# A third staging buffer, a new order of VectorE's additions, and residual additions on GpSimd, in a fused attention and mixer kernel

## The reference

```python
x  = attention(q, k, v)             # 4 batches, 576 tokens, 8 heads x 64, window 128
u  = x + (x^T @ U @ V)^T            # tokens mixed through rank 32: "the mixed tokens"
x2 = u + relu(u @ w_ch1) @ w_ch2    # w_ch1 512x2048, w_ch2 2048x512
# then a gated unit: relu(x2 @ w_in), layer norm, spatial product, gate, @ w_out
```

## Time and profile before

| what | value |
|---|---|
| median of 3 runs | 742.33 us (742.27 to 743.06) |
| the profiled execution | 742.42 us |
| its span, first to last instruction | 740.6 us |
| TensorE matmul busy | 719.5 us, 97% of the span |
| weight load busy | 664.1 us, 90% |
| VectorE busy | 457.0 us, 62% |
| ScalarE busy | 339.2 us, 46% |
| GpSimd busy | 182.0 us, 25% |

### The profile page before, as it was taken

How to read it: one execution, slowest core, us unless ns; L and a number is a source line. 1 busy time by engine, 2 the same in 40 slices (tenths; PEclk the granted TensorE clock), 3 DMA queues, 4 the chain that set the end, 5 groups by cost and what they waited for, 6 DMA issues and landing times.

```text
span 740.6 us, 13178 instructions
## 1 busy us (share of the span) xinstructions
PE 719.5 (97%) x4688; PEld 664.1 (90%) x4688; DVE 457.0 (62%) x1032; ACT 339.2 (46%) x764; POOL 182.0 (25%) x183
## 2 busy tenths in 40 slices
PE   7999999999999999989899999999999999999998
PEld 5777777689989989989799999999899998998997
DVE  6878787788763365226977885986365435444331
ACT  5977777854452243224344444445262432432422
POOL 1597546520007873353041000000010100100100
PEclk9999999999999999999999999999999999999999
DMA  6569954046446864798976454667820100100101
GB/s 207 185 232 394 336 207 136 16 150 206 170 147 239 285 248 164 233 385 312 428 253 195 146 166 136 193 222 264 304 108 1 54 12 0 64 0 0 64 0 65
DMA packets 74066, 128.24 MB, mean 173 GB/s; under 512 B 5024, under 2 KB 44960, under 8 KB 73504
## 3 DMA queue, kind: packets, MB, share of 16 engines
q1 hardware_dynamic: 74016, 127.59, 49.4%
HBM read 76.91 MB, written 50.66 MB: 172 GB/s over the span
## 4 chain that ended last, share of the span: by engine, by line
PE 61%; DVE 8%; DMA 4%; issue 3%; POOL 2%; ACT 1%; SPq 0%; DVEq 0%; POOLq 0%; ACTq 0%
PE bank L1881 5%; PE bank L1883 5%; PE bank L1882 5%; PE bank L1923 4%; PE bank L1925 4%; PE bank L1924 4%; PE bank L2032 2%; PE bank L2034 2%; PE bank L2033 2%; PE bank L1846 2%; PE bank L1848 2%; PE bank L1847 2%; PE wide L1847 2%; PE wide L1846 2%; PE wide L1848 2%
## 5 line engine op out<-in xcount | busy, mean ns | idle before, releaser
L1881 PE MATMUL bank<-xs,w1s 128*128 128x384 f32 x336 | 114.2, 340 | 7.4 <-DVE tok L1414 4.0
L1883 PE MATMUL bank<-xs,w1s 128*128 128x384 f32 x336 | 113.0, 336 | 0.0
L1882 PE MATMUL bank<-xs,w1s 128*128 128x384 f32 x336 | 113.0, 336 | 0.0
L1055 ACT ACTIVATE rk<-tok 128x768 fp32r<-128x768 f32 x72 | 60.8, 848 | 77.8 <-PE bank L1925 35.6
L901 POOL TENSOR_TENSOR vl<-vr,vh 128x512 fp32r<-128x512 f32 x8 | 11.3, 1407 | 293.5 <-ACT vh L1179 293.5
L1038 ACT ACTIVATE sums_u<-bank 128x384 f32<-128x384 f32 x72 | 35.4, 492 | 99.2 <-PE bank L1883 90.1
L914 ACT ACTIVATE sc<-sc,mn 128x256 f32<-128x256 f32 (+1 forms) x144 | 67.0, 468 | 20.4 <-DVE mn L1239 20.3
L1923 PE MATMUL bank<-rk,w2q 128*128 128x384 f32 x208 | 70.5, 339 | 4.0 <-DVE rk L1436 2.3
L1881 PEld LDWEIGHTS bank<-xs,w1s 128*128 128x128 f32 x336 | 63.5, 189 | 10.4 <-DVE tok L1414 5.3
L1924 PE MATMUL bank<-rk,w2q 128*128 128x384 f32 x208 | 69.5, 334 | 0.0
L1925 PE MATMUL bank<-rk,w2q 128*128 128x384 f32 x208 | 69.5, 334 | 0.0
(11 more groups left out here) (220 smaller groups left out, 1847.8 us busy)
## 6 DMA issues: line engine op xcount, KB each, us to landing
r_scr<-tok SPq DMA_DIRECT2D x18, 768.0 KB, 4.3
tok<-r_scr SPq DMA_DIRECT2D x18, 768.0 KB, 7.6
qkraw<-qk SPq DMA_DIRECT2D x32, 288.0 KB, 4.0
w1raw<-w SPq DMA_DIRECT2D x32, 256.0 KB, 3.6
w2q<-w_scr SPq DMA_DIRECT2D x4, 2048.0 KB, 13.9
wc_scr<-wprep SPq DMA_DIRECT2D x12, 512.0 KB, 6.0
w_scr<-tok SPq DMA_DIRECT2D x11, 512.0 KB, 2.8
u_scr<-tok SPq DMA_DIRECT2D x6, 768.0 KB, 4.4
```

The source lines that it names most:

```text
L1055: act.activation(rk[:, n % RING, 0], raw(g, RAW_OF[m])[:, 2 * j:2 * j + 2, :], ACT.Relu if m <= 3 else ACT.Copy).then_inc(rk_hi, 1)
L1881: pe.matmul(o, wh, ah, start=(k == 0 and m in FRESH), stop=False, skip_group_check=True)
L1882: pe.matmul(o, wl, ah, start=False, stop=False, skip_group_check=True)
L1883: last = pe.matmul(o, wh, al, start=False, stop=(k == 1), skip_group_check=True)
```

## The change

Six edits, all in the second stage:

1. Step 22 stages its blocks in a new buffer `late2`, with a semaphore `r_last` of its own for its store, and waits for no earlier store. `late2` covers the third slot of the ring `rk`, so `hi_r(2)` waits for `r_last` and moves behind the last `keep_p`. The load of `raw_c` no longer waits for the store of step 22. Steps 18 to 21 and 23 use `late0` and `late1` as before.
2. At a change of group `c12(s-1)` goes ahead of `x_sum(g+1, 2)` and of the low parts 5 and 7; `c11` and `c22` of the last step change places; ScalarE does `hi_xs(g+1, 1)` ahead of `c21`, and `hi_xs(g, 7)` after `hi_xs(g, 5)`; `X_ORDER` has 5 ahead of 7. `relu_b(s-1)` now stands behind `lo_xs(g, 5)` and `lo_xs(g, 7)` in step u = 0.
3. At the start `c22(0)` goes ahead of `w1_sum_of(2)` (four additions of 128x256).
4. In `SUMS[0]` the sums (3,0) and (2,0) move up to entry (1,3), and the rest follows by one place.
5. `add_res` moves from VectorE to GpSimd, for all groups, in one loop that stands behind `split_direct(4)`.
6. `dc21` of groups 0 and 1 is done two entries later.

```diff
-X_ORDER = [1, 2, 6, 7, 5, 4, 3]
+X_ORDER = [1, 2, 6, 5, 7, 4, 3]
...
+LATE_AT = {18: 0, 19: 1, 20: 0, 21: 1, 22: 2, 23: 1}
...
-    0: {(2, 0): [(3, 0), (2, 0)], (2, 1): [(3, 1), (2, 1)], (2, 2): [(3, 2), (2, 2)], (2, 3): [(3, 3), (2, 3)],
-        (6, 0): [(4, 0), (1, 0)], (6, 1): [(4, 1), (1, 1)], (6, 2): [(4, 2), (1, 2)], (6, 3): [(4, 3), (1, 3)]},
+    0: {(1, 3): [(3, 0), (2, 0)], (2, 0): [(3, 1), (2, 1)], (2, 1): [(3, 2), (2, 2)], (2, 2): [(3, 3), (2, 3)],
+        (2, 3): [(4, 0)], (6, 0): [(4, 1), (1, 0)], (6, 1): [(4, 2), (1, 1)], (6, 2): [(4, 3), (1, 2)],
+        (6, 3): [(1, 3)]},
...
+        pl.enter_context(nc.sbuf_tensor("gap9", [P, 7168], F32))
+        late += [sb(pl, "late2", [P, 4, HT], F32)]
...
-                return late[s % 2][:, n, :]
+                return late[LATE_AT[s]][:, n, :]
...
-                sp.dma_start(r_scr[g, u], r_stage(s)).then_inc(r_out[s % 2], 16)
+                sp.dma_start(r_scr[g, u], r_stage(s)).then_inc(r_last if s == 22 else r_out[s % 2], 16)
...
-            sp.wait_ge(r_out[0], 16 * NU // 2)
+            sp.wait_ge(r_out[0], 16 * (NU // 2 - 1))
             load_raw(0, "c", 0)
             load_raw(0, "c", 1)
             store_r(NU - 1)
...
             sp.wait_ge(r_out[1], 16 * NU // 2)
+            sp.wait_ge(r_last, 16)
             load_u(0, 11)
...
             pool.wait_ge(rk_used, DN_AT[(0, 5)])
             split_direct(4)
 
+            def add_res(g, n):
+
+                kept, done, i = {11: (dp1_kept, dp1_u, 0), 12: (du2_kept, du2_u, 1), 22: (du3_kept, du3_u, 2)}[n]
+                pool.wait_ge(u_back[0 if n in (11, 22) else 1], 32 * g + (16 if n != 22 else 32))
+                for m in range(2):
+                    pool.wait_ge(kept, 2 * g + m + 1)
+                    o = sums_d[:, i, m]
+                    pool.tensor_tensor(o, o, u_in[:, 0 if n in (11, 22) else 1, m], ALU.add).then_inc(done, 1)
+
+            for g in range(G):
+                add_res(g, 11)
+                add_res(g, 12)
+                add_res(g, 22)
...
-                if s >= 2:
+                if s >= 2 and s != 22:
                     act.wait_ge(r_out[s % 2], 16 * (s // 2))
...
+                if n == 2:
+                    act.wait_ge(r_last, 16)
...
+                if u == UNITS - 1 and g < G - 1:
+                    hi_xs(g + 1, 1)
                 c21(s - 1)
...
                 if u == 0:
                     hi_xs(g, 5)
+                    hi_xs(g, 7)
                     hi_xs(g, 4)
                 if u == UNITS - 1 and g < G - 1:
-                    hi_xs(g + 1, 1)
                     hi_xs(g + 1, 2)
                 if s == NU - 1:
-                    for n in range(RING):
+                    for n in range(2):
                         hi_r(n)
...
                 keep_p(s, 7)
-                if u == UNITS - 1 and g < G - 1:
-                    hi_xs(g + 1, 7)
+            hi_r(2)
...
             c11(0)
+            c22(0)
             w1_sum_of(2)
-            c22(0)
...
                 if u == 0:
                     x_sum(g, 1)
-                    lo_xs(g, 7)
...
                 if last:
                     lo_xs(g + 1, 1)
-                    x_sum(g + 1, 2)
+                c12(s - 1)
                 if u == 0:
                     lo_xs(g, 5)
-                c12(s - 1)
+                    lo_xs(g, 7)
                 relu_b(s - 1)
+                if last:
+                    x_sum(g + 1, 2)
...
                     x_sum(g + 1, 4)
-                    c22(s)
...
                 c11(s)
                 if last:
+                    c22(s)
                     lo_xs(g + 1, 6)
...
-                if ended[2] == DP - 1 and ended[1] in (2, 3, 4) and ended[0:2] != (0, 2):
-                    g, m = ended[0:2]
-                    dc21(g) if m == 4 else dc(g, 11 if m == 2 else 12)
-                ended = ENTRIES[n - RING - 1] if n > RING else (0, 0, 0)
-                if ended[2] == DP - 1 and ended[1] in (1, 6, 7) and ended[0:2] not in ((0, 1), (0, 6)):
-                    add_res(ended[0], {1: 11, 6: 12, 7: 22}[ended[1]])
+                if ended[2] == DP - 1 and ended[1] in (2, 3) and ended[0:2] != (0, 2):
+                    dc(ended[0], 11 if ended[1] == 2 else 12)
+                elif ended == (G - 1, 4, DP - 1):
+                    dc21(G - 1)
+                if n > DP and ENTRIES[n - DP - 1][1:] == (4, DP - 1) and ENTRIES[n - DP - 1][0] < G - 1:
+                    dc21(ENTRIES[n - DP - 1][0])
                 if n == ENTRY[(0, 7)]:
-                    add_res(0, 11)
                     dc(0, 11)
-                elif n == ENTRY[(0, 7)] + 1:
-                    add_res(0, 12)
```

More of the change, by code:

```diff
@@ L251, in program @@
         r_out = [sem(f"r_out{i}") for i in range(2)]
+        r_last = sem("r_last")
         w2_out = [sem(f"w2_out{i}") for i in range(3)]
@@ L1457, in r_sum @@
                                              op1=ALU.subtract).then_inc(rt1, 1)
[L1459 to L1466, removed]
             def dc(g, n):
```

## The result

| | before | after |
|---|---|---|
| median | 743.06 us (742.27 to 743.14, 5 runs) | 750.55 us (750.07 to 751.64, 5 runs) |
| the profiled execution | 742.42 us, span 740.6 | 751.64 us, span 749.8 |

The ratio is 1.0105, 95% interval [1.0091, 1.0119]: slower by 7.5 us, where 6.9 were forecast.

What follows compares the result with a forecast made beforehand. TensorE, with a matmul in flight for 97% of the span, was taken as the bound; 742.4 - 0.3 - 1.9 - 2.8 + 0.8 - 0.4 + 11.7 + 1.7 - 1.9 = 749.3, as a median 749.2 us, range 746.4 to 753.

Steps and rivals of the forecast that it cites:

- Edit 5: Ahead of product (0,7): TensorE stands while GpSimd's additions wait behind `split_direct(4)`, 11.7 us lost, bounds 10.9 to 14.4.
- Rival D: Ahead of (0,7): no stall, because GpSimd reaches the additions before TensorE runs dry; 735.8 us, chance 0.03.
- rival A: At the stall: split keeps its 10.6, clock stays low twice as long, or group 1's data is late; 753 us, chance 0.08.
- The clock behind the stall: After the stall ahead of (0,7): the granted clock falls and costs 1.7 us, bounds 0 and 3.4.
- Edit 2, second change: At the second change of group: 1.9 plus 0.9 of a 1.1 wait won, 2.8 us in all.
- the last of the prediction's own signs of being wrong: In the up phase: its first waits come back further on in another place, as at the start; no size given.
- rival B: At the changes of group: GpSimd's weight work slows VectorE, so the won time doesn't come; 751.7 us, chance 0.09.
- Edit 3: Start of the up phase: 1.45 us won at `c22(0)`, but `up(1, 5)` then waits; 0.3 us stay, bound 1.4.
- The wait at `up(21, 3)`: At `up(21, 3)`: not removed; grows by 0.8 us because `relu_b(15)` ends later behind two low parts.
- Edits 1 and 4: Sums of group 0: first sum starts at 349.1 instead of 350.4; 0.4 us won, bounds 1.9 and -0.7.
- the clock at 325 us: Behind the wait at `up(21, 3)`: 3.5 us at half clock cost 1.7 us, and that stays.
- rival C: Whole kernel: edits end nearly all VectorE waits, the 2.3 and the clock's 1.7 at 325 us included; 740.8 us, chance 0.04.

Runs made afterwards that it cites:

- e1: The kernel after, but GpSimd does `add_res(0, 11)` and `add_res(0, 12)` ahead of its wait for product (0,5) and of `split_direct(4)`: 738.78 us.
- e2: The kernel after, but additions 11 and 12 of group 0 stand in the middle of `split_direct(4)`, two of its four pairs ahead of them: 747.46 us.
- e4: The kernel before with only `add_res` moved to GpSimd behind `split_direct(4)`: 756.83 us, ratio 1.0192 to before.
- f7: f1, but GpSimd's `split_w2(5)` works on 8 of 256 columns, with as many instructions and signals: 735.9 us in one run.
- f3: f1, but `relu_b(s-1)` stands ahead of `lo_xs(g, 5)` and `lo_xs(g, 7)` again: 735.17 us, ratio 0.9895 to before.
- f1: e1, but GpSimd waits for the end of product (0,6) before `add_res(0, 11)` and `add_res(0, 12)`: 737.05 us, ratio 0.9919 to before.

## Why the prediction was right

**Edit 5: right, in mechanism and size.** TensorE is idle for 11.53 us, where about 11.4 were named. Each term of the stall against the trace after: the split 7.64 (7.9), each addition 0.98 (1.0), the second half of `dc` 0.56 (0.5), `lo_r` 1.19 by the chain (0.95), with GpSimd's third addition beside it. Together with 0.27 for signals and the restart that is 11.62, where 11.7 were forecast. e1 and e2 show the cause by moving only the place in the queue; e4 shows that it needs none of the other edits. Rival D, no stall, is out. Of rival A the dear split is out: 7.64 with VectorE standing, and 10.56 for the same eight instructions in e1 (380.28 to 390.84), where VectorE works beside them for 6.40 us. The DMA queues, which also stood still in the stall, don't explain the pair: `split_direct(1)` took 7.87 in the kernel before at a DMA share of 1.04, with VectorE busy for 2.11. The Trainium skill ("SBUF — State Buffer", section "Who interferes with whom") says that a VectorE instruction with two SBUF inputs and a GpSimd instruction that reads SBUF shut each other out, and these numbers agree. It holds in the other direction too: VectorE's sums at 0.95 and at 2.05 in f7 and after. Rival A's late data of group 1 is out as well: TensorE has no wait row between (1,1) and the end of the down phase.

**The clock behind the stall: right, on thin ground.** 1.92 against 1.7; I took the figure from the one example at hand, so that its size came out is partly luck. The clock fell during the stall, not after it, and what it cost is the 3.9 us of work until 393.5.

**Edit 6: right.** 0.96 and 0.92, against 0.95.

**Edit 2, first change: right.** 1.86 against 1.9, and no wait row left.

**Edit 2, second change: mis-sized, and this is the term of the sum that failed.** "0.9 of 1.1 is won ... 2.8 at the second" took the durations of the undisturbed first change (there GpSimd is idle for 64.86 us, until 223.33). Of 2.8 only 0.8 came: 1.8 was won at `up(15, 5)`, but 1.3 came back at `up(15, 3)`, where TensorE now waits for `c22(15)`: a wait that comes back further on, which is the last of the prediction's own signs of being wrong. f7 shows why: GpSimd's `split_w2(5)` runs in that very stretch, doubles VectorE's sums, and without it the stretch is as short as the first. This is rival B's mechanism, which I had at 0.09, and the rows of before had it: two waits of 1.9 and 1.1 there against 1.0 and 1.1 at the first change, for the same instructions. I had named the cause in the rival and left it out of the sum.

**Edit 3: mis-sized the other way.** Forecast -0.3, measured -0.8. The wait did move on, as said, but with 0.52 idle at 165.16 in place of the 1.18 at 159.44.

**The wait at `up(21, 3)`: the mechanism right, the size off.** It grew by 0.22 and not 0.8; f3 shows that `relu_b`'s place feeds it, since the wait shrinks by 1.7 when that is taken back. On VectorE's timelines `relu_b(15)` starts 0.02 us ahead of TensorE's `up(16, 5)` before, 0.64 behind it after, and 1.57 ahead of it in f3; from there to `up(21, 3)` it is 43.2, 42.8 and 43.2 us. So 0.66 of the 0.8 was there, and 0.46 came back in the chain of DMAs behind it; what shortened that chain isn't shown.

**Edits 1 and 4, and the clock at 325 us: near in the sum, wrong in the parts.** Forecast -0.4, measured -0.15 (46.70 to 46.55 us from `up(21, 3)` to (0,5)). Inside, TensorE stands 3.31 us for `hi_r(2)`, where before it didn't stand (ScalarE is idle for 7.0 us until the store has landed), and then little for the sums: waits of 1.0 to 0.2 us ahead of eight entries before, of 0.35 to 0.2 ahead of three after. "3.5 us at 0.51 cost 1.7. That stays" was wrong twice: the half clock moved from 325 to 345 us, and by the table under f3 such a stretch costs nothing at the end in any of its five kernels, all with the third buffer. So rival C's 1.7 us for the clock weren't there to be won.

So the forecast was near (6.9 against 7.5) partly by errors that offset one another in part: against 2.0 us too much at the second change stand 0.5 too little won at the start and 0.6 too much lost at `up(21, 3)`. Stage by stage the profile gives 8.3 and not 7.5, which is 1.4 over the forecast; that the medians lie nearer is luck as far as these runs can tell.

## What to carry to other kernels

When an instruction moves to another engine, ask first what stands ahead of it in that engine's queue and what that waits for: here 2 us of additions cost 13 because a split that waits for TensorE stood ahead of them, and nothing that could be measured when moved up past it and out of VectorE's full stretch (f1). Price a stretch by rows of the same stretch, with the same neighbours: beside each other VectorE's sums took up to 2.2 times and GpSimd's additions 1.6 times their time, so an idle engine isn't free. And an instruction that starts a chain of DMAs (`relu_b`) goes ahead of work that only has to be done in time.

## What the hardware showed unexpectedly

The clock's fall behind a short wait isn't told by the wait's length. After the wait at `up(21, 3)` it fell in the kernel before with 1.99 us idle, and stayed at full in after with 2.21; behind `hi_r(2)` it fell in f1 with 3.12 us idle and stayed in f3 with 3.16. What decides between them no run here shows. And whether the fall costs anything isn't told by its length either: 1.9 us behind the stall, nothing between `up(21, 3)` and (0,5), where VectorE and the store were the bound, though TensorE worked for most of it.

GpSimd's addition of 128x384 took 0.98 us with VectorE standing, but 1.14 in the mean of 18, beside 0.55 on VectorE. The group by line, after:

```profile
L910 POOL TENSOR_TENSOR sums_d<-sums_d,u_in 128x384 f32<-128x384 f32 x18 | 20.1, 1140 | 105.5 <-ACT sums_d L1087 53.9
```
